# Moving the z sums of a linear attention to another PSUM bank and slot, and one gate step in the layer behind it

## The chip, the cores and the metric

The kernel runs on one core of a Trainium2 chip. The metric is the device time of one execution in microseconds. The kernel before takes 821.87 us, the median of three runs (821.83 to 821.92).

## The reference

The work is a linear attention, then a gated layer, then a layer of eight experts of which each token takes one. Constants of shape: 4 batches, 8 heads, 576 positions, 64 channels a head, 128 features; 2304 tokens of 512 channels; hidden widths 2048 and 1024.

```python
def phi(x):                                   # 64 -> 128 -> 256 features
    proj = x @ w_phi
    proj = proj - max(abs(proj), axis=-1)
    return concatenate([exp(proj), exp(-proj)], axis=-1)
q_p, k_p = phi(q), phi(k)
kv = k_p.T @ v                                # per head, 256 x 64
z = sum(k_p, axis=positions)                  # per head, 256
x = (q_p @ kv) / (q_p @ z + 1e-6)             # numerators, denominators

h = x @ w_in                                  # 2304 x 2048
g = h * clip(h + 3, 0, 6) / 6
x = g @ w_out

e = argmax(x @ w_gate)                        # one of 8 experts a token
out = gate * sigmoid(x @ w_output_gate)[e] * (relu(x @ w1[e]) @ w2[e])
```

## The kernel before

Everything is one program with an instruction list written out by hand for each engine; the engines meet in semaphores. Nothing is planned at build time: the order of the calls in the functions below is the order of the work.

**Attention** takes the 32 heads in 16 pairs. Each engine has a function `both(u, a)` for pair `u` (`a` is its parity, for double buffers), unrolled for the first and last pairs and looped between; `last_pair` ends it. From the eighth pair on (the second half, `phase` 1) ScalarE and VectorE also scale the pieces of w_in and w_out into two float16 parts; before that, VectorE searches them for their maximum. The steps of a pair are:

- TensorE projects q and k tiles of the next pair in three groups (`projections`, line 749: tiles of 64 rows; group 0 is one tile, groups 1 and 2 are four).
- VectorE searches maxima, subtracts them for q and negates them for k (`differences`).
- ScalarE makes the exponentials of k (`k_features`, line 1144) and, behind TensorE's transposes (line 765), those of q (`q_features`, line 1127).
- TensorE sums kv over positions into PSUM bank KVB (line 781), ScalarE copies it (`copy_kvt`, line 1156), TensorE turns it (`kv_transposes`, line 790), ScalarE copies it again (`copy_kv`, line 1162).
- GpSimd adds the k features of all tiles (`sums_first`, `sums_second`, lines 596 and 612), five additions; its result `pk_summed` goes to TensorE's `z_sums` (line 799: four tiles of 32 columns), then ScalarE's `copy_z_rows` (line 1168), TensorE's `z_transpose` (line 805), ScalarE's `copy_z` (line 1174).
- TensorE makes the low and high numerators (line 812, tiles of 64 columns, banks NB and NB + 1) and the denominators (line 821, tiles of 32 columns, both banks). ScalarE copies the low bank (`copy_low`, lines 1180 and 1181), VectorE the high one (`copy_high`).
- The denominators go through DRAM to get turned and spread: SP issues `den_over`, VectorE takes reciprocals, SP issues `rec_out` and `rec_in`, GpSimd multiplies (`normalise`, line 616).

The banks: KVB is 0, NB is 6, KB is (3, 5). In the kernel before z rows and z stand in bank KVB behind kv. In two pairs (`top`) a maximum over partitions is also found (`max_turn`, `max_over`, lines 828 and 832).

SP's queue issues the loads of q and k (`next_qk`), of v (`next_v`, four DMAs), of weight pieces (`next_pieces`, two DMAs) and the three steps of the denominators, in the order of the loop at line 454. A step that waits holds up all that are behind it.

**The gated layer** takes the tokens in 6 blocks of 384, and each block in 16 column chunks `f` of the hidden width. Per chunk: TensorE's `hidden` (line 925, 12 matmuls), ScalarE's relu (line 1284), VectorE's product (`gate_chunk`, line 1684), ScalarE's high half of the gate (line 1295, semaphore `g_hi`), VectorE's low half (`gate_lo`, line 1689, semaphore `g_ready`), TensorE's `output` (line 936, 9 matmuls). TensorE works two chunks ahead: `hidden(f + 2)`, then `output(f)`. Between these steps VectorE and ScalarE prepare the expert weights in units: per unit VectorE searches four quarters for their maximum in two steps (line 1606), reduces it (line 1610), GpSimd reduces over partitions (line 646), VectorE makes the scale (lines 1621 to 1624), ScalarE scales the quarters (line 1272), VectorE makes their low halves (line 1631). In `mlp_block` of VectorE the first unit's second search is at chunk 3, its scale at chunk 4, its first low halves at chunk 5. In ScalarE's `mlp_block` the first quarter follows the gate's half of chunk 4 and stands ahead of the relu of chunk 5; the second follows that relu, ahead of the wait for the product.

Where `gate_lo` of a chunk stands is set by one line: for chunks in `SOON` it comes right behind `gate_chunk`, for all others at the end of the chunk's work:

```python
SOON = (0, 1, 2, FC - 1)            # line 69, FC = 16
...
gate_chunk(n, f)                    # lines 1732 to 1734
if f in SOON:
    gate_lo(n, f)
...
if j == 2 and 0 <= k < units:       # line 1757, k, j = divmod(f - 1, 5)
    unit_search(n * 3 + k, (a + k) % 2, 2)
...
if f not in SOON and not (post and f == Y_AT + 9 - ahead):
    gate_lo(n, f)                   # line 1775
```

**The experts** follow in slots of 128 tokens (lines 1026 and 1038).

## Time and profile before

| | us |
|---|---|
| median of three runs | 821.87 |
| profiled execution | 821.83 |
| its span | 820.2 |
| attention, to about | 182 |
| gated layer, to about | 563 |

```profile
PE 802.9 (98%) x7080; PEld 498.6 (61%) x7081; DVE 558.2 (68%) x1144; ACT 390.8 (48%) x863; POOL 182.7 (22%) x210
PE   9999999999999999999999999999999999999995
DVE  6788798878988988988898897845723453222221
ACT  6888888884655654754645646534101121010110
POOL 4456666660000011010010001010311232111000
PEclk9999999999999999999999999999999999999998
PE 58%; DVE 18%; issue 12%; ACT 8%; DMA 2%; POOL 1%; DVEq 0%; POOLq 0%; ACTq 0%
```

The first line gives each engine's busy time, its share of the span and its instructions. PE is TensorE's matmuls, PEld its loads of weights, which overlap them, DVE is VectorE, ACT ScalarE, POOL GpSimd. The next lines cut the span into 40 equal slices of 20.5 us; a digit is the busy share in tenths, and for PEclk the granted clock of TensorE. Attention is the first nine slices, the gated layer goes to slice 27. The last line is the chain that ended last, by engine. A busy TensorE means that matmuls were in flight, not that they ran at their best rate.

### The profile page before, as it was taken

The page shows a single profiled execution, that of the slowest core. Times are in us where ns is not written, and L with a number is a line of the kernel's source. Part 1 is how long each engine was busy: PE and PEld are TensorE (multiplying, and loading weights), DVE is VectorE, ACT ScalarE, POOL GpSimd, SP SyncE. Part 2 cuts the span into 40 slices and gives each one's busy share as a digit, 9 for nine tenths or more (in the row PEclk, how much of TensorE's full clock was granted, in tenths as well). Part 3 has the DMA queues.
Part 4 walks back from the last instruction along what each step waited for, and adds up shares of the span by engine and source line. Part 5 has one row for each costly group of instructions (what it writes and reads, how often), then busy time and mean ns, then how long its engine had stood idle before and what let it go on. Part 6 is the DMA issues. An engine that isn't in the chain of part 4 may idle for free.

```text
span 820.2 us, 19346 instructions
## 1 busy us (share of the span) xinstructions
PE 802.9 (98%) x7080; PEld 498.6 (61%) x7081; DVE 558.2 (68%) x1144; ACT 390.8 (48%) x863; POOL 182.7 (22%) x210
## 2 busy tenths in 40 slices
PE   9999999999999999999999999999999999999995
PEld 7666666655555555555555555556777777777773
DVE  6788798878988988988898897845723453222221
ACT  6888888884655654754645646534101121010110
POOL 4456666660000011010010001010311232111000
PEclk9999999999999999999999999999999999999998
DMA  8566778736557657765765766394274926166600
GB/s 254 182 199 219 213 202 243 217 110 220 220 205 225 225 216 237 240 227 208 218 246 179 245 217 198 135 343 145 85 278 164 361 64 256 61 242 240 237 27 15
DMA packets 67454, 164.41 MB, mean 200 GB/s; under 512 B 28614, under 2 KB 32966, under 8 KB 60736
## 3 DMA queue, kind: packets, MB, share of 16 engines
q1 hardware_dynamic: 61472, 146.74, 52.9%
q0 software_dynamic: 5760, 16.80, 5.8%
q8 instruction: 36, 0.59, 0.3%
q14 instruction: 26, 0.21, 0.1%
q10 hardware_dynamic: 160, 0.07, 0.0%
HBM read 114.16 MB, written 47.55 MB: 197 GB/s over the span
## 4 chain that ended last, share of the span: by engine, by line
PE 58%; DVE 18%; issue 12%; ACT 8%; DMA 2%; POOL 1%; DVEq 0%; POOLq 0%; ACTq 0%
PE ps L936 11%; PE ps L1026 11%; PE ps L1038 11%; PE ps L925 10%; DVE u_mx L1606 4%; DVE arena L1631 4%; PE ps L749 3%; ACT arena L1144 3%; PE ps L781 3%; DVE relu L1684 2%; PE ps L812 2%; DVE y_words L1598 2%; DVE arena L1356 1%; DVE stage L1689 1%; PE ps L765 1%
## 5 line engine op out<-in xcount | busy, mean ns | idle before, releaser
L925 PE MATMUL ps<-arena,w_in_sb 128*128 128x384 f16 x1152 | 200.9, 326 | 0.0
L936 PE MATMUL ps<-w_out_sb,arena 128*128 128x512 f16 x576 | 171.3, 379 | 1.8 <-DVE stage L1689 1.8
L925 PEld LDWEIGHTS ps<-arena,w_in_sb 128*128 128x128 f16 x1152 | 111.9, 98 | 81.1 <-issue 0.2
L1323 ACT ACTIVATE x_t<-ps 128x512 f16<-128x512 f32 x54 | 31.6, 596 | 198.7 <-PE ps L1026 173.4
L1026 PE MATMUL ps<-x_t,arena 128*128 128x128 f16 x2112 | 121.5, 219 | 1.3 <-issue 1.3
L1026 PEld LDWEIGHTS ps<-x_t,arena 128*128 128x128 f16 x2112 | 119.2, 98 | 5.1 <-issue 1.8
L1038 PE MATMUL ps<-arena,x_t 128*128 128x512 f16 x528 | 117.9, 379 | 0.0
L936 PE MATMUL ps<-w_out_sb,stage 128*128 128x512 f16 x288 | 109.1, 379 | 0.0
L1295 ACT ACTIVATE arena<-relu 128x384 f16<-128x384 f32 x96 | 50.0, 521 | 122.6 <-DVE relu L1684 122.4
L936 PEld LDWEIGHTS ps<-w_out_sb,arena 128*128 128x128 f16 x576 | 55.9, 98 | 61.8 <-issue 4.6
L1797 DVE SCALAR_TENSOR_TENSOR x_t<-ps,x_t 128x512 f16<-128x512 f32 x54 | 36.7, 689 | 77.8 <-ACT x_t L1323 77.8
L1144 ACT ACTIVATE arena<-ps,arena 128x128 f32<-128x128 f32 x288 | 81.5, 416 | 9.7 <-DVE arena L1353 9.7
L1038 PEld LDWEIGHTS ps<-arena,x_t 128*128 128x128 f16 x528 | 50.6, 98 | 56.7
L596 POOL TENSOR_TENSOR arena<-arena 128x512 f32<-128x512 f32 (+1 forms) x64 | 69.2, 1081 | 59.6 <-ACT arena L1144 55.5
L1631 DVE SCALAR_TENSOR_TENSOR arena<-arena,u_up 128x1024 f16<-128x1024 f32 x64 | 79.3, 1280 | 3.7 <-ACT arena L1272 3.7
L1284 ACT ACTIVATE relu<-ps,three,s_h 128x384 f32<-128x384 f32 x96 | 63.5, 662 | 38.0 <-PE ps L925 37.4
L1272 ACT ACTIVATE arena<-arena,u_up 128x1024 f16<-128x1024 f32 x64 | 72.5, 1140 | 6.2 <-DVE u_up L1623 6.2
L1606 DVE TENSOR_REDUCE u_mx<-arena 128x1 f32<-128x1024 f32 x64 | 74.8, 1210 | 0.0
L646 POOL PARTITION_ALL_REDUCE u_all<-u_red x16 | 7.8, 490 | 290.9 <-DVE u_red L1610 290.9
L1684 DVE SCALAR_TENSOR_TENSOR relu<-relu,ps 128x384 f32<-128x384 f32 x96 | 52.7, 549 | 26.3 <-ACT relu L1284 24.6
L1807 DVE TENSOR_SCALAR x_t<-ps,stage 128x512 f32<-128x512 f32 x27 | 20.2, 748 | 68.5 <-PE ps L1038 68.5
L1689 DVE SCALAR_TENSOR_TENSOR stage<-relu,arena 128x384 f16<-128x384 f32 x96 | 53.1, 553 | 19.4 <-ACT arena L1295 19.2
(210 smaller groups left out, 912.8 us busy)
## 6 DMA issues: line engine op xcount, KB each, us to landing
arena<-split SPq DMA_DIRECT2D x36, 1024.0 KB
arena<-in_moe_w SPq DMA_DIRECT2D x16, 2048.0 KB, 12.8
split<-arena SPq DMA_DIRECT2D x16, 2048.0 KB, 7.4
arena<-in_qkt SPq DMA_DIRECT2D x15, 576.0 KB, 4.2
stage<-in_moe_w_in SPq DMA_DIRECT2D x16, 512.0 KB, 4.4
stage<-in_moe_w_out SPq DMA_DIRECT2D x16, 512.0 KB, 5.7
x_t<-rows POOLq DMA_DIRECT2D x27, 257.0 KB
y_words<-recs SPq DMA_DIRECT2D x32, 144.0 KB, 3.9
```

The lines of the kernel that those rows point to most:

```text
L596: nc.gpsimd.tensor_tensor(out, x, y, ALU.add).then_inc(sum_step, 1)
L925: last = nc.tensor.matmul(ps[:, HB[f % GB], 0:BN], w_in_sb[:, lw, c, f * P:(f + 1) * P], xt[:, a, lx, c, :], start=c == 0 and lw + lx == 0 ...
L936: last = nc.tensor.matmul(ps[:, YB + r, :], g_sb[lg_][:, f % GB, r * P:(r + 1) * P], w_out_sb[:, lw, f, :], start=f == 0 and lg_ + lw == 0 ...
L1026: last = nc.tensor.matmul(ps[:, bank, f % 4 * P:(f % 4 + 1) * P], w1_sb[b][:, lw, c, f * P:(f + 1) * P], xgt[:, a, lx, c, :], start=c == 0 ...
L1038: last = nc.tensor.matmul(ps[:, 6 + a, :], hg[:, a, lh, f, :], w2_sb[b][:, lw, f, :], start=f == 0 and lh + lw == 0, stop=f == EFC - 1 and ...
L1144: last = nc.scalar.activation(pk[:, t0 + t, s, :], ps[:, bank, t * F:(t + 1) * F], ACT.Exp, bias=bias[:, t0 + t:t0 + t + 1], scale=1.0 - 2 ...
L1272: nc.scalar.activation(split_sb[:, 0, q_ * Q:(q_ + 1) * Q], raw[b][:, q_ * Q:(q_ + 1) * Q], ACT.Copy, scale=u_up[:, b:b + 1]).then_inc(u_h ...
L1284: nc.scalar.activation(relu3[:, f % GB, :], ps[:, HB[f % GB], 0:BN], ACT.Relu, bias=three[:, 0:1], scale=s_h[:, 0:1]).then_inc(relu3_ready, 1)
L1606: nc.vector.tensor_reduce(u_mx[:, q_:q_ + 1], raw[b][:, q_ * Q:(q_ + 1) * Q], AX.X, ALU.max, apply_absolute_value=True).then_inc(u_searche ...
L1631: nc.vector.scalar_tensor_tensor(out=split_sb[:, 1, cols], in0=raw[b][:, cols], scalar=u_up[:, b:b + 1], in1=split_sb[:, 0, cols], op0=ALU ...
L1684: nc.vector.scalar_tensor_tensor(out=relu3[:, f % GB, :], in0=relu3[:, f % GB, :], scalar=6.0, in1=ps[:, HB[f % GB], 0:BN], op0=ALU.min, o ...
L1689: nc.vector.scalar_tensor_tensor(out=g_sb[1][:, f % GB, :], in0=relu3[:, f % GB, :], scalar=CG / 6.0, in1=g_sb[0][:, f % GB, :], op0=ALU.m ...
```

## The change

In attention the z rows and z move from bank KVB to bank NB + 1 (in the last pair to bank 3), which the high numerators overwrite. TensorE makes the z sums ahead of the low numerators, turns z right behind them, and waits for the copy of z ahead of the high numerators; the wait of the denominators goes. ScalarE's `both` has k features of group 0 ahead of `copy_kv` and `copy_low`, and makes both z copies before the next pair's k features of group 1, no longer in their midst. SP issues values and reciprocals ahead of the weight pieces, and reciprocals one pair sooner. In the gated layer chunk 3 joins `SOON`.

```diff
--- before.py
+++ after.py
@@ -66,7 +66,7 @@
 USTEPS = 4
 Y_AT = 3
 UNIT_AT = 1
-SOON = (0, 1, 2, FC - 1)
+SOON = (0, 1, 2, 3, FC - 1)
 W_UP = 3
 YSTEPS, YUP = 6, 4
 ONEHOT, ARGS, ROUTE = 7, 9, 19
@@ -332,11 +332,12 @@
 
 
         QB, KB, TB, KVB, NB = 4, (3, 5), (1, 2), 0, 6
-        DEN_AT, ZR_AT, Z_AT = LOW, 2 * F, 2 * F + P
+        DEN_AT, ZR_AT, Z_AT = LOW, 0, F
         TOPS, MAX_AT = (PAIRS // 2 - 1, PAIRS - 2), DEN_AT + QUARTER
         KQ, RUN = (1, 0), (7, 6)
         FIRST = (TB[::-1], (NB, NB + 1), (QB, KB[0]))
         WEIGHTS, VALUES = (0, 3), (1, 1)
+        Z_LAST = KB[0]
 
         YB, HB, XB, LB = 0, (3, 4, 5), 6, 7
         TURNED, AHEAD = (6, 7, 1, 4), 2
@@ -452,14 +453,14 @@
 
             next_qk(2)
             for u in range(PAIRS):
-                if u > 3:
-                    rec_in(u - 4)
                 if u > 2:
                     rec_out(u - 3)
+                if u + 2 < PAIRS:
+                    next_v(u + 2)
+                if u > 2:
+                    rec_in(u - 3)
                 if 0 < u < PAIRS - 1:
                     next_pieces(u - 1)
-                if u + 2 < PAIRS:
-                    next_v(u + 2)
                 if u > 0:
                     den_over(u - 1)
                 if u + 3 < PAIRS:
@@ -484,7 +485,6 @@
                 sp.dma_start(split[bass.ds(e, 1), m, :, :].rearrange("o p n -> (o p) n"),
                              split_sb.rearrange("p l n -> p (l n)")).then_inc(u_stored, 16)
 
-            rec_in(PAIRS - 4)
             sp.wait_ge(num_done, PAIRS)
             load_unit(0, 0, 0)
             rec_out(PAIRS - 3)
@@ -790,19 +790,21 @@
                     last = nc.tensor.transpose(ps[:, KVB, s * P:s * P + P], kvt_sb[:, s, :], ident[:])
                 last.then_inc(kv_transposed, 1)
 
-            def z_sums(u):
+            def z_sums(u, bank=NB + 1):
 
                 pe.wait_ge(pk_summed, u + 1)
+                if bank == NB + 1 and (not isinstance(u, int) or u > 0):
+                    pe.wait_ge(high_copied, u)
                 for s in range(2):
                     for hh in range(2):
                         g = REP * (2 * s + hh)
-                        last = nc.tensor.matmul(ps[g:g + REP, KVB, ZR_AT:ZR_AT + F], ones[:, 0:REP], pk_sum[:, hh, s, :],
+                        last = nc.tensor.matmul(ps[g:g + REP, bank, ZR_AT:ZR_AT + F], ones[:, 0:REP], pk_sum[:, hh, s, :],
                                                 start=True, stop=True)
                 last.then_inc(z_summed, 1)
 
-            def z_transpose(u):
+            def z_transpose(u, bank=NB + 1):
                 pe.wait_ge(zr_ready, u + 1)
-                nc.tensor.transpose(ps[:, KVB, Z_AT:Z_AT + P], zr_sb, ident[:]).then_inc(z_turned, 1)
+                nc.tensor.transpose(ps[:, bank, Z_AT:Z_AT + P], zr_sb, ident[:]).then_inc(z_turned, 1)
 
             def numerators(bank, k, n, signs=(0, 1)):
 
@@ -841,20 +843,20 @@
                 dif_transposes(u, a, 2)
                 kv_transposes(u)
                 projections(u + 1, 1 - a, 1)
+                z_sums(u)
                 pe.wait_ge(kv_ready, u + 1)
                 pe.wait_ge(pq_ready, u * 3 + 2)
                 if not isinstance(u, int) or u > 0:
                     pe.wait_ge(low_copied, u)
                 numerators(NB, 0, LOW)
-                z_sums(u)
+                z_transpose(u)
                 projections(u + 1, 1 - a, 2)
-                z_transpose(u)
+                if top == VALUES:
+                    max_turn(*top)
                 pe.wait_ge(pq_ready, u * 3 + 3)
-                if not isinstance(u, int) or u > 0:
-                    pe.wait_ge(high_copied, u)
+                pe.wait_ge(z_ready, u + 1)
                 numerators(NB + 1, LOW, HIGH)
-                pe.wait_ge(z_ready, u + 1)
-                if top is not None:
+                if top == WEIGHTS:
                     max_turn(*top)
                 last = denominators()
                 if top is not None:
@@ -875,11 +877,11 @@
                 pe.wait_ge(low_copied, u)
                 numerators(NB, 0, LOW)
                 pe.wait_ge(pk_ready, u * 3 + 3)
-                z_sums(u)
+                z_sums(u, Z_LAST)
                 pe.wait_ge(pq_ready, u * 3 + 3)
                 pe.wait_ge(high_copied, u)
                 numerators(NB + 1, LOW, HIGH, (0,))
-                z_transpose(u)
+                z_transpose(u, Z_LAST)
                 numerators(NB + 1, LOW, HIGH, (1,))
                 pe.wait_ge(z_ready, u + 1)
                 denominators().then_inc(num_done, 1)
@@ -1129,7 +1131,7 @@
                                                 scale=1.0 - 2.0 * s)
                 last.then_inc(pq_ready, 1)
 
-            def k_features(u, a, g, between=None):
+            def k_features(u, a, g):
                 t0, n = GROUPS[g]
                 act.wait_ge(neg_ready, u * 3 + (g + 1))
                 if g == 0 and (not isinstance(u, int) or u > 0):
@@ -1145,8 +1147,6 @@
                                                     bias=bias[:, t0 + t:t0 + t + 1], scale=1.0 - 2.0 * s)
                     if g == 2 and t == 2:
                         last.then_inc(pk_half, 1)
-                    if between is not None and t == 1:
-                        copy_z(between)
                 last.then_inc(pk_ready, 1)
 
             def copy_kvt(u):
@@ -1161,17 +1161,17 @@
                     act.wait_ge(num_done, u)
                 nc.scalar.copy(kv_sb[:].rearrange("p s n -> p (s n)"), ps[:, KVB, 0:2 * P]).then_inc(kv_ready, 1)
 
-            def copy_z_rows(u):
+            def copy_z_rows(u, bank=NB + 1):
                 act.wait_ge(z_summed, u + 1)
                 if not isinstance(u, int) or u > 0:
                     act.wait_ge(z_turned, u)
-                nc.scalar.copy(zr_sb, ps[:, KVB, ZR_AT:ZR_AT + F]).then_inc(zr_ready, 1)
-
-            def copy_z(u):
+                nc.scalar.copy(zr_sb, ps[:, bank, ZR_AT:ZR_AT + F]).then_inc(zr_ready, 1)
+
+            def copy_z(u, bank=NB + 1):
                 act.wait_ge(z_turned, u + 1)
                 if not isinstance(u, int) or u > 0:
                     act.wait_ge(num_done, u)
-                nc.scalar.copy(z_sb[:].rearrange("p s h n -> p (s h n)"), ps[:, KVB, Z_AT:Z_AT + P]).then_inc(z_ready, 1)
+                nc.scalar.copy(z_sb[:].rearrange("p s h n -> p (s h n)"), ps[:, bank, Z_AT:Z_AT + P]).then_inc(z_ready, 1)
 
             def copy_low(u, a):
                 act.wait_ge(num_done, u + 1)
@@ -1203,13 +1203,14 @@
                 q_features(u, 0)
                 q_features(u, 1)
                 copy_kvt(u)
+                k_features(u + 1, 1 - a, 0)
+                copy_kv(u)
                 if not isinstance(u, int) or u > 0:
                     copy_low(u - 1, 1 - a)
-                copy_kv(u)
-                k_features(u + 1, 1 - a, 0)
+                copy_z_rows(u)
                 q_features(u, 2)
-                copy_z_rows(u)
-                k_features(u + 1, 1 - a, 1, between=u)
+                copy_z(u)
+                k_features(u + 1, 1 - a, 1)
                 if phase:
                     piece_hi_of(u, a)
 
@@ -1226,8 +1227,8 @@
                 copy_low(u - 1, 0)
                 copy_kv(u)
                 q_features(u, 2)
-                copy_z_rows(u)
-                copy_z(u)
+                copy_z_rows(u, Z_LAST)
+                copy_z(u, Z_LAST)
                 piece_hi_of(u, 1)
                 copy_low(u, 1)
                 nc.scalar.activation(wg_sb[:, 0], wg_raw[:], ACT.Copy, scale=s_up[:, 2:3]).then_inc(wg_hi, 1)
```

## Rows read from the trace of the kernel before

**Rows 1.** The waits of TensorE: line, what it waited for, us, times, longest.
```profile
PE ps L936 <- DVE stage L1689: 1.8, 5, 0.6
```

**Rows 2.** Windows: length; busy PE, PEld, DVE, ACT, POOL (x count); clock; DMA share; GB/s.
```profile
67.08:77.75 10.67, 10.67 (x126) 6.80 (x124) 8.66 (x18) 8.71 (x30) 6.63 (x7) 1.00 0.66 214
111.28:122.20 10.92, 10.79 (x124) 6.80 (x125) 9.82 (x20) 9.69 (x32) 7.51 (x7) 1.00 0.80 229
```

**Rows 3.** Time line before denominators: start us, us, instruction [idle before <-releaser].
```profile
71.51 1.08 PE L812 MATMUL ps<-arena 128*64 128x256 f32 x8
...
71.94 0.28 ACT L1174 COPY arena<-ps 128x128 f32<-128x128 f32 x1
...
72.52 0.89 PEld L821 LDWEIGHTS ps<-arena 128*32 128x32 f32 x32 [0.39 <-ACT arena L1174]
```

**Rows 4.** The time line at the low numerators, first half.
```profile
66.98 1.27 POOL L612 TENSOR_TENSOR arena<-arena 128x512 f32<-128x512 f32 x1
...
68.54 1.30 PE L812 MATMUL ps<-arena 128*64 128x320 f32 x8
```

**Rows 5.** The waits of ScalarE, at the copy of z rows.
```profile
ACT arena L1168 <- PE ps L799: 12.9, 16, 0.8
```

**Rows 6.** The time line of the first pair.
```profile
14.32 1.27 POOL L612 TENSOR_TENSOR arena<-arena 128x512 f32<-128x512 f32 x1
...
15.16 1.30 PE L812 MATMUL ps<-arena 128*64 128x320 f32 x8
```

**Rows 7.** The time line of one pair of the second half.
```profile
111.28 0.20 PEld L790 LDWEIGHTS ps<-ident,arena 128*128 128x128 f32 x2 [0.37 <-ACT arena L1156]
...
111.65 1.16 PE L749 MATMUL ps<-wphi_sb,arena 64*128 64x128 f32 x16
...
115.12 1.14 ACT L1144 ACTIVATE arena<-ps,arena 128x128 f32<-128x128 f32 x4 [0.40 <-DVE arena L1353]
...
117.55 5.10 POOL L596 TENSOR_TENSOR arena<-arena 128x512 f32<-128x512 f32 x4 [3.10 <-ACT arena L1144]
...
122.72 1.27 POOL L612 TENSOR_TENSOR arena<-arena 128x512 f32<-128x512 f32 x1
```

**Rows 8.** The time line of block 1, chunks 2 to 4.
```profile
255.76 0.56 DVE L1689 SCALAR_TENSOR_TENSOR stage<-relu,arena 128x384 f16<-128x384 f32 x1 [0.59 <-ACT arena L1295]
...
261.40 0.55 DVE L1689 SCALAR_TENSOR_TENSOR stage<-relu,arena 128x384 f16<-128x384 f32 x1
261.66 0.49 POOL L646 PARTITION_ALL_REDUCE u_all<-u_red  x1 [26.56 <-DVE u_red L1610]
261.86 0.55 DVE L1684 SCALAR_TENSOR_TENSOR relu<-relu,ps 128x384 f32<-128x384 f32 x1
...
262.09 0.59 PE L936 MATMUL ps<-w_out_sb,arena 128*128 128x512 f16 x2 [0.26 <-DVE stage L1689]
...
263.59 1.15 ACT L1272 ACTIVATE arena<-arena,u_up 128x1024 f16<-128x1024 f32 x1 [0.63 <-DVE u_up L1623]
```

**Rows 9.** The time line at chunk 5 of blocks 0, 1, 2 and 5.
```profile
206.32 0.55 DVE L1689 SCALAR_TENSOR_TENSOR stage<-relu,arena 128x384 f16<-128x384 f32 x1
...
207.17 0.59 PE L936 MATMUL ps<-w_out_sb,arena 128*128 128x512 f16 x2
...
268.78 0.55 DVE L1689 SCALAR_TENSOR_TENSOR stage<-relu,arena 128x384 f16<-128x384 f32 x1
...
269.87 0.38 PE L936 MATMUL ps<-w_out_sb,arena 128*128 128x512 f16 x1
...
332.48 0.56 DVE L1689 SCALAR_TENSOR_TENSOR stage<-relu,arena 128x384 f16<-128x384 f32 x1
...
333.27 0.59 PE L936 MATMUL ps<-w_out_sb,arena 128*128 128x512 f16 x2
...
522.48 0.55 DVE L1689 SCALAR_TENSOR_TENSOR stage<-relu,arena 128x384 f16<-128x384 f32 x1
...
523.75 0.59 PE L936 MATMUL ps<-w_out_sb,arena 128*128 128x512 f16 x2
```

## The prediction

> **What bounds the kernel now.** I read three views, in this order. First the waits of TensorE: it is idle hardly anywhere, and the largest entry is five waits of up to 0.6 us for VectorE's line 1689, the low half of the gate [rows 1]. Then the windows over one head pair of attention: 10.67 us in the first half, 10.92 us in the second [rows 2]. TensorE is busy for all of the first and for all but 0.13 us of the second, so in attention it is the bound, or within 0.25 us of it. Last the time line around each place that the diff touches, to see how much earlier than needed each semaphore comes. The profiled execution took 821.83 us, with a span of 820.2 us; that is 0.04 under the median of 821.87, so I add the changes to 821.83 and call the rest the same.
>
> **The attention part, costs of the instructions.** No matmul, copy or activation is added or removed: the four z sums, the z transpose and their two copies move, to another bank and another place. TensorE shows a gap of 0.39 us ahead of the denominators' weights, for which it names the copy of z [rows 3]. If that gap were the wait, merging it into the one ahead of the high numerators would pay. But the copy ends at 71.94 + 0.28 = 72.22, 0.30 before the weights at 72.52. What the gap costs beyond the streaming: eight matmuls go in four couples from 71.51 to 72.59; with 0.38 for one, the last couple starts at 72.21 and the couples are 0.23 apart, so a next one was due at 72.44, 0.08 before 72.52. I count these 0.08 us as the price of going from 128x64 to 128x32 tiles, not of the wait. The order before has the shapes projection, numerators, z sums, projection, z transpose, numerators, denominators; the order after has projection, z sums, numerators, z transpose, projection, numerators, denominators: six changes each. So I take 0; the bounds are 0 and a gain of 16 x 0.08 = 1.3 us. The Trainium skill (TensorEngine Tiling (Array Packing), Key Properties) says that changing the tiling mode drains TensorE, while a change of tile alone does not. By it the sum stays at 0 here; by the other reading it would fall by 1.3 us.
>
> **The z sums now come 1.2 us earlier, and wait for GpSimd.** They stood behind the low numerators; now they take the numerators' slot, right behind the second projections. That slot opens at 68.54, 1.46 us behind the pair's start at 67.08 [rows 2, 4]. GpSimd ends the sums of features (line 612) at 66.98 + 1.27 = 68.25 [rows 4], so in the first half there is 0.29 us to spare. The other waits that move (for the low and high halves of the pair before, and for z) cost nothing there either: ScalarE stood idle for 0.8 us a pair at the z rows (12.9 us in 16 waits [rows 5]) and takes the copies into that time. So 0 for seven pairs; with that idle time gone, the low copy's pass would be late by at most as much.
>
> Not so in the first pair. GpSimd ends its sum at 14.32 + 1.27 = 15.59, the slot opens at 15.16 [rows 6]. With 0.07 us for the semaphore the z sums start at 15.66: **+0.50 us**. TensorE is the bound behind it, so this is not given back. Bounds 0.3 to 0.6.
>
> **Second half.** What ends last is now ScalarE: TensorE idles before the kv transposes for the copy of kv (the 0.37) [rows 7], which is the 0.25 us between the two windows [rows 2]. ScalarE's loop is k features, z copy, a weight piece, more k and q features, kv copy. The z copy leaves it for ScalarE's idle time. It has a duration of 0.28 us [rows 3], but the queue's instructions overlap; I take half, 0.14, bounds 0 and 0.28. ScalarE's loop would then allow 10.92 - 0.14 = 10.78 us.
>
> But the z sums need GpSimd. From the second projections of a pair (111.65 [rows 7]) to the first activation of the next pair's k features (115.12) are 3.47 us; from there to GpSimd's start (117.55) 2.43, now 2.29 without the z copy; GpSimd's five additions take from 117.55 to 122.72 + 1.27 = 123.99, which is 6.44 us; the semaphore 0.07. So z sums of a pair start no earlier than 12.27 us behind the second projections of the pair before. And from the z sums to the next pair's second projections TensorE needs 10.67 us less the way from projections to slot, 1.46 - 0.37 = 1.09 (0.37 is 111.28 to 111.65), so 9.58 us. Two pairs therefore take at least 12.27 + 9.58 = 21.85 us, **10.93 us a pair**, against 10.92 before. The wait for kv goes and a wait for GpSimd of about 0.25 us at the z sums takes its place. With the entry into this phase I take **+0.1 us** for the half. Bounds: -1.0 (seven times 0.14, GpSimd not binding) and +3.1: GpSimd works 7.51 us in a pair of this half and 6.63 in one of the first [rows 2], 0.88 more, because one of its additions meets a VectorE pass over a weight piece; a second meeting would cost two pairs 0.88, one pair 0.44, seven pairs 3.1. The Trainium skill (GPSIMD Engine Reference, Specifications) has GpSimd's memory interface in contention with VectorE instructions with two SBUF inputs. That is the kind of pass meant here, so it bears on the upper bound alone.
>
> **The DMA queue.** SP now issues the values' four loads and the two loads of reciprocals ahead of the two weight pieces. The pieces so leave later by six issues. A piece is read by VectorE only in the second pair behind its issue, so a whole pair, 10.67 us [rows 2], lies between; 0. If that lead were gone, VectorE would stand at a piece, and the projections behind it.
>
> **The gated blocks: line 69 (SOON).** For column chunk 3 of each block the low half of the gate is made right behind the product, no longer behind VectorE's second search of a weight unit. These are the five waits of rows 1, each at chunk 3 of blocks 1 to 5. At the old place it ran at once, 261.40, and kept VectorE 0.46 us until the next product at 261.86. At the new one it has to wait for ScalarE's half, which starts only when the product is done: in chunk 2, where this order already stands, VectorE idles 0.59 and works 0.56 [rows 8], 1.15 us together. All that follows is late by 1.15 - 0.46 = **0.69 us**, and that is the unit's scale (line 1621). GpSimd's maximum, which the scale also needs, is there at 261.66 + 0.49 = 262.15, 1.44 before ScalarE's first quarter at 263.59 [rows 8]; between them lie only VectorE's product and its own short steps, so it does not hide the delay.
>
> From the scale on it is a chain without slack: ScalarE's first quarter waits for the scale (0.63 us idle for line 1623) [rows 8], its relu of chunk 5 stands behind that quarter, VectorE's product behind the relu, ScalarE's next quarter, VectorE's two passes over quarters, and last the low half of chunk 5. So the latter is late by 0.69 us. TensorE's output matmul starts 0.14 us behind the end of such a half when it waits for it (261.40 + 0.55 = 261.95, then 262.09) [rows 8]. That gives, for chunk 5 [rows 9]:
> block 0: 206.32 + 0.55 + 0.69 + 0.14 = 207.70, before 207.17: +0.53;
> block 1: 268.78 + 0.55 + 0.83 = 270.16, before 269.87: +0.29; block 3 has the same distances;
> block 2: 332.48 + 0.56 + 0.83 = 333.87, before 333.27: +0.60; block 4 likewise;
> block 5: 522.48 + 0.55 + 0.83 = 523.86, before 523.75: +0.11.
> The removed wait at chunk 3 is already in these: TensorE arrives earlier at chunk 5 and waits there instead. Sum 0.53 + 2 x 0.29 + 2 x 0.60 + 0.11 = **+2.42 us**. From chunk 6 on the halves come early enough. Bounds: +2.9 (0.1 us more in each of five blocks) and, without the chain, the -1.8 us of the waits [rows 1].
>
> **Sum.** 0.50 + 0.1 + 2.4 = 3.0 us: 821.83 + 3.0 = **824.8 us**.
>
> **The rivals.**
> *A, faster: the delay ends before TensorE.* Place: chunk 5. If VectorE's later work absorbs the 0.69 us, only the removed waits at chunk 3 count, -1.8 us, and with the first pair +0.5 and the second half between -1.0 and +0.1 the time is 819.5 to 820.6. It decides as soon as the low half of chunk 5 is late by less than 0.2 us in block 0 and on time in block 2, since these have no slack: in block 0 the half ends at 206.87, and 0.14 later is 0.16 before the start at 207.17. For it: the waits of rows 1 are real. Against it: no idle time in the chain that I can find but the ones counted.
> *B, GpSimd does not bind:* ScalarE's 10.78 rules, second half -1.0: 823.7. Or the gap before the denominators was the wait, -1.3: 823.5. For it: 0.15 us a pair decides between the loops. Against: by the sum above GpSimd ends 0.5 us behind the slot at the shorter rhythm (12.27 against 10.67 + 1.09 = 11.76).
> *C, GpSimd meets VectorE twice:* +3.1, 827.9.
> *D, parts cancel:* half of A's effect, the time within 1.6 us of before.
>
> **How the numbers follow.** Chances: my forecast 0.58 (own range 824.0 to 826.0), B 0.13, C 0.05, A 0.16, D 0.08. 0.2% is 1.64 us, about what can be told from no change. Faster by more than that needs A with the better attention, and A's edge lies on it: 0.15. D and the rest of A: 0.11. Slower: 0.74. The range 820.7 to 826.4 leaves out A's better half and C, and a little on each side.
>
> **What would show it.** In the trace of after: the z sums of the first pair idle until GpSimd at 15.66; pairs of 10.67 us, then of 10.93, with the wait for the kv copy gone and one for line 612 in its place; no wait at chunk 3, but five or six at chunk 5 that name line 1689, of 0.3 to 1.0 us; the denominators' gap as before. I am wrong on the sign if chunk 5 shows none, and wrong in the attention part if the pairs of the second half take 10.8 us or less.

## The result: slower by 0.7%, and the profile after

| | before | after |
|---|---|---|
| median of the executions timed side by side, us | 821.83 | 825.88 |
| spread of these five | 820.69 to 821.92 | 824.88 to 828.56 |
| ratio, 95% interval | | 1.0069 (1.0046 to 1.0094) |
| profiled execution, us | 821.83 | 828.33 |
| its span, us | 820.2 | 826.7 |
| attention, to about | 181.8 | 184.8 |
| gated layer, its length | 381.1 | 384.1 |
| experts, their length | 247.5 | 248.0 |

The kernel after is slower, by 3.8 to 7.7 us (the interval times 821.83). Its executions lie further apart than those of before: with the profiled one and two more (829.33 and 829.37) the median of all eight is 827.6, and the ratio fits these eight. The profiled one lost 3.0 us in attention, 3.0 in the gated layer and 0.5 behind it.

The page after: busy time, VectorE and granted clock in 40 slices, and the chain that ended last.

```profile
PE 802.4 (97%) x7080; PEld 497.4 (60%) x7081; DVE 557.6 (67%) x1144; ACT 394.2 (48%) x863; POOL 183.6 (22%) x210
DVE  6788789877978988898897897845622453222221
PEclk9999999999999999999999999999999999999998
PE 53%; DVE 21%; issue 11%; ACT 5%; DMA 5%; POOL 3%; SPq 1%; DVEq 0%; ACTq 0%; POOLq 0%
```

The matmuls take what they took (802.4 us against 802.9) at the same clock, so the loss is idle time of TensorE. The chain shows whose: DMA has grown from 2% to 5% of it, VectorE from 18% to 21%. TensorE's waits name the places (line, what it waited for, us, times, longest); the first answers to [rows 1], the others had no row among them:

```profile
PE ps L938 <- DVE stage L1690: 4.5, 7, 1.1
PE ps L834 <- DVE s_row L1437: 2.4, 2, 1.7
PE ps L801 <- POOL arena L612: 1.4, 6, 0.4
PE ps L790 <- ACT arena L1156: 0.7, 2, 0.3
```

Lines have moved by a few: 938 is the output, 1690 the gate's low half, 834 the maximum over partitions, 801 the z sums, 790 the kv transposes. The windows over one pair of the first half, one of the second, and the last two full pairs (length; busy PE, PEld, DVE, ACT, POOL; clock; DMA share; GB/s) answer to [rows 2]:

```profile
67.02:77.67 10.65, 10.65 (x127) 6.80 (x125) 8.68 (x18) 8.96 (x31) 6.63 (x7) 1.00 0.69 205
122.07:132.96 10.89, 10.71 (x126) 6.80 (x124) 9.54 (x19) 10.01 (x32) 7.50 (x7) 1.00 0.72 227
154.77:166.23 11.46, 10.91 (x126) 6.76 (x124) 9.40 (x19) 10.03 (x32) 8.06 (x7) 1.00 0.67 208
166.23:179.75 13.52, 11.16 (x125) 6.88 (x125) 10.30 (x21) 9.90 (x32) 9.23 (x8) 1.00 0.60 171
```

Behind the first pair the windows have the lengths that were forecast, 10.65 and 10.89, up to 154.77. Then two pairs take 0.5 and 2.6 us more than the 10.92 they took before: this is the loss in attention. The chain of waits through them (start us, us, what; a wait on a transfer stands at its issue):

```profile
154.87 7.71 DMA recs<-rec
162.59 0.46 SPq L434
...
163.74 0.58 SPq L396
...
164.36 7.57 DMA stage<-in_moe_w_out
171.93 0.02 issue
171.95 0.76 DVE w_in_sb L1420
```

SP stores the reciprocals at 154.87, and the next step in its queue is now the load of the same reciprocals (`rec_in(u - 3)`, line 434). It stands there until the store has landed, 7.71 us, with the two weight pieces behind it. They are issued at 163.74 and 164.36, and the later one lands at 171.93, when VectorE has been standing at it for 1.9 us (the other 0.8 us of the row belong to the pair before):

```profile
DVE w_in_sb L1420 <- DMA stage<-in_moe_w_out: 2.7, 2, 1.9
```

In the trace of before, SP issued the same two right behind the store:

```profile
152.39 0.33 SPq L417 DMA_DIRECT2D recs<-rec  x1
154.30 0.34 SPq L395 DMA_DIRECT2D stage<-in_moe_w_in  x1
154.68 0.44 SPq L398 DMA_DIRECT2D stage<-in_moe_w_out  x1
```

In the gated layer the time line of block 1, chunks 2 to 4, answers to [rows 8]:

```profile
261.98 0.55 DVE L1685 SCALAR_TENSOR_TENSOR relu<-relu,ps 128x384 f32<-128x384 f32 x1
...
263.12 0.56 DVE L1690 SCALAR_TENSOR_TENSOR stage<-relu,arena 128x384 f16<-128x384 f32 x1 [0.59 <-ACT arena L1296]
...
267.80 1.15 ACT L1273 ACTIVATE arena<-arena,u_up 128x1024 f16<-128x1024 f32 x1 [0.63 <-DVE u_up L1624]
```

Chunk 3's low half (263.12) idles VectorE for 0.59 us as foreseen. ScalarE's first quarter starts at 267.80, against 263.59 before. VectorE's products up to chunk 3 are 3.49 us behind the trace of before, so the quarter is 267.80 - 263.59 - 3.49 = 0.72 us late; 0.69 was forecast. Chunk 5 of blocks 0, 1 and 2 [rows 9], and chunk 15 of block 1:

```profile
210.66 0.59 PE L938 MATMUL ps<-w_out_sb,arena 128*128 128x512 f16 x2 [0.37 <-DVE stage L1690]
...
273.69 0.59 PE L938 MATMUL ps<-w_out_sb,arena 128*128 128x512 f16 x2 [0.58 <-DVE stage L1690]
...
309.70 0.59 PE L938 MATMUL ps<-w_out_sb,arena 128*128 128x512 f16 x2 [0.18 <-DVE stage L1690]
...
338.13 0.59 PE L938 MATMUL ps<-w_out_sb,arena 128*128 128x512 f16 x2 [1.02 <-DVE stage L1690]
```

The row at 309.70 had not been foreseen. Pairing the 96 outputs and the 96 VectorE products (line 1685) of both traces in order gives how far each is behind the trace of before, in us:

| block | TensorE at its end | VectorE's products, chunks 4 to 15 | chunk 5 added (forecast) | chunk 15 added |
|---|---|---|---|---|
| 0 | 3.49 | 3.64, then 3.49 from chunk 11 | 0.53 (0.53) | 0 |
| 1 | 4.15 | 4.20 to 4.22 | 0.32 (0.29) | 0.34 |
| 2 | 4.86 | 4.92 to 4.95 | 0.71 (0.60) | 0 |
| 3 | 5.73 | 5.79 to 5.81 | 0.53 (0.29) | 0.34 |
| 4 | 6.33 | 6.38 to 6.45 | 0.60 (0.60) | 0 |
| 5 | 5.97 | 7.02, then 6.45 from chunk 9 | 0.11 (0.11) | -0.48 |

"Added" is net of the wait at chunk 3 that goes. The two columns sum to 2.80 and 0.20, and 2.95 (attention) + 3.00 is the 5.97 at the end, within rounding. In blocks 1 to 4 VectorE does not catch up once in twelve chunks: it hands its lateness on.

### The profile page after: what moved, and what is told of

It is laid out like the page before. It is cut to its first block, busy times and chain, and to the rows that moved or that the text cites. A ratio compares the mean times of both kernels' runs of the same rounds, so it can differ in the third digit from the quotient of the medians.

```text
span 826.7 us, 19359 instructions
## 1 busy us (share of the span) xinstructions
PE 802.4 (97%) x7080; PEld 497.4 (60%) x7081; DVE 557.6 (67%) x1144; ACT 394.2 (48%) x863; POOL 183.6 (22%) x210
## 4 chain that ended last, share of the span: by engine, by line
PE 53%; DVE 21%; issue 11%; ACT 5%; DMA 5%; POOL 3%; SPq 1%; DVEq 0%; ACTq 0%; POOLq 0%
PE ps L1028 11%; PE ps L1040 11%; PE ps L938 10%; PE ps L927 9%; DVE u_mx L1607 5%; DVE arena L1632 4%; DMA recs<-rec 3%; PE ps L749 2%; DVE relu L1685 2%; PE ps L781 2%; PE ps L814 2%; DVE stage L1690 2%; POOL arena L596 2%; ACT arena L1296 2%; DMA stage<-in_moe_w_out 2%
## 5 line engine op out<-in xcount | busy, mean ns | idle before, releaser
L596 POOL TENSOR_TENSOR arena<-arena 128x512 f32<-128x512 f32 (+1 forms) x64 | 71.0, 1109 | 60.1 <-ACT arena L1146 55.9
L1146 ACT ACTIVATE arena<-ps,arena 128x128 f32<-128x128 f32 x288 | 79.1, 399 | 7.8 <-DVE arena L1354 7.8
```

The costliest lines, as they stand in the source:

```text
L596: nc.gpsimd.tensor_tensor(out, x, y, ALU.add).then_inc(sum_step, 1)
L1146: last = nc.scalar.activation(pk[:, t0 + t, s, :], ps[:, bank, t * F:(t + 1) * F], ACT.Exp, bias=bias[:, t0 + t:t0 + t + 1], scale=1.0 - 2 ...
```

## The experiments

Each is compared with executions of the kernel before on the same chip (medians 821.56 to 821.81). The diffs are against the kernel named.

**Three parts, taken apart.** First the kernel after with SyncE's old order:

```diff
+                if u > 3:
+                    rec_in(u - 4)
                 if u > 2:
                     rec_out(u - 3)
-                if u + 2 < PAIRS:
-                    next_v(u + 2)
-                if u > 2:
-                    rec_in(u - 3)
                 if 0 < u < PAIRS - 1:
                     next_pieces(u - 1)
+                if u + 2 < PAIRS:
+                    next_v(u + 2)
...
+            rec_in(PAIRS - 4)
```

> The kernel after, with SP's order of issues as before the change (weight pieces ahead of the values, reciprocals loaded four pairs behind). Theory 1 (the loss in attention comes from SP, which now waits in line for the store of reciprocals, 7.7 to 7.9 us, and so issues the last weight pieces 9.6 us late): pairs 14 and 15 return to 10.9 us or less, attention ends about 3 us sooner, 3 us less than after in all, near 824 us, and with little spread between runs. Theory 2 (the loss comes from the earlier maximum matmul of pair 14 or from the ordering of the z sums): pair 14 still waits 1.7 us for line 1437 and the time stays near that of after. The wait at chunk 5 stays in both.

Measured 825.53 (824.51 to 826.23), ratio 1.0052 (1.0038 to 1.0066). Attention ends at 181.2 in its trace, the gated layer takes 383.9. In the profiled executions the 3 us of attention come and go with SyncE's order. In the timings it was not yet told: 825.53 is more than the expected 824, the five times of after run from 824.88 up, the lowest lie among these, and the two intervals overlap.

The kernel after without `3` in SOON:

```diff
-SOON = (0, 1, 2, 3, FC - 1)
+SOON = (0, 1, 2, FC - 1)
```

> The kernel after, with chunk 3 out of SOON again. Theory 1 (low half of chunk 3 made early delays the low half of chunk 5 by 0.69 us): the six waits ahead of the output of chunk 5 go, five waits at chunk 3 of up to 0.6 us return, and the gated blocks are 2.4 to 3.0 us shorter than in after. Rival (the gated blocks are longer because weights or reciprocals arrive later from the new DMA order): the waits stay and the time too.

Measured 822.41 (820.78 to 825.36, 11 executions), ratio 1.0016 (1.0006 to 1.0026). The gated layer is back at 380.9, and attention, with SyncE's new order, ends at 181.6.

The kernel before with `3` in SOON and nothing else:

> The kernel before, with chunk 3 in SOON and nothing else. Theory 1: +2.4 us by the sum of the prediction, up to +3.0 by the trace of after; waits of 0.3 to 1.0 us ahead of the output of chunk 5 in all six blocks. Rival (it costs only together with the rest of the change): between -1.8 and 0.

Measured 824.65 (824.24 to 825.12), ratio 1.0039 (1.0026 to 1.0053): +3.2 us, 2.1 to 4.4. The gated layer takes 383.9. TensorE's wait is that of after:

```profile
PE ps L936 <- DVE stage L1689: 4.6, 8, 1.0
```

The kernel before with SyncE's new order and nothing else:

> The kernel before, with SP's order of issues as after and nothing else. Theory 1: about +3 us, all of it in pairs 13 to 15, with the last weight pieces issued 8 to 10 us later than before and VectorE waiting for them; more spread between runs, since the store's round trip varies. Theory 2 (SP's order is harmless without the moved z sums): within 0.5 us of before.

Measured 821.74 (820.64 to 822.76, 11 executions), ratio 1.0001 (0.9992 to 1.001). SyncE waits 40.4 us for its stores (49.9 in after, below), and it costs nothing here. That SyncE's order adds 3 us whenever it is there has fallen with this run. What was left: it costs only where the weight pieces come so late that their lead is used up, which happens in some executions and not in others.

```profile
SPq L433 <- DMA recs<-rec: 40.4, 11, 7.9
```

**The bank and the order on TensorE and ScalarE alone** (the change without its edits to SyncE and SOON):

> The kernel before with the first part of the change alone: the z tensors in their own bank, z sums and z transpose moved forward on TensorE, and ScalarE's copies moved with them. SyncE's order and SOON stay as before. My theory: this part is worth next to nothing. From the trace of after, the first pair costs 0.2 us, the six pairs of the second half take 10.90 us each instead of 10.92, and the first half 10.645 instead of 10.68 (6 x 0.035 = 0.2 us gained): sum about 0, time 821.4 to 822.0. The prediction had +0.6 (822.4). Rival: the part gains more and is hidden in after by the other two; then 820.8 to 821.2. In the list of waits, z sums <- GpSimd appears about six times with a mean of 0.4 us, and output <- VectorE with four or five of chunk 3, as before.

Measured 822.19 (821.7 to 824.6, 11 executions), ratio 1.001 (1.0001 to 1.0019): 0.1 to 1.6 us slower, between the two expectations, with the prediction's +0.6 inside. A window over a pair of the second half has the length of after, and in TensorE's waits the one for GpSimd is there six times:

```profile
133.03:143.96 10.93, 10.71 (x126) 6.81 (x124) 9.72 (x19) 9.97 (x32) 7.57 (x7) 1.00 0.83 230
```

```profile
PE ps L802 <- POOL arena L613: 1.3, 6, 0.4
```

**The same with GpSimd's last addition cut short:**

```diff
-                nc.gpsimd.tensor_tensor(pk_sum[:], pk_sum[:], pk[:, 5:8:2], ALU.add).then_inc(pk_summed, 1)
+                nc.gpsimd.tensor_tensor(pk_sum[:, :, :, 0:8], pk_sum[:, :, :, 0:8], pk[:, 5:8:2, :, 0:8], ALU.add).then_inc(pk_summed, 1)
```

> The same kernel with GpSimd's fourth addition for the z sums cut to 8 of its columns (the denominators then leave out most of four of the nine feature tiles' last term). If z sums wait for GpSimd in the second half, as the prediction's first two terms have it, the wait of about 0.25 us over the fixed 0.2 us goes in each pair of the second half: period 10.64 to 10.70 instead of 10.90, 6 x 0.25 = 1.5 us, and 0.2 us in the first pair: 1.5 to 1.7 us under the kernel with this part alone. Rival: the kv copy, whose wait was 0.156 us a pair before, is late again behind it, or VectorE's queue sets the period; then 0 to 0.6 us under it.

The whole time, 831.85, is not to be compared: the denominators change, with them the routing, and the experts take 258.5 us instead of 247.8. Attention can be compared. A window over a pair of its second half takes 10.75 us. In the time line of the same pair GpSimd's last addition is done in 0.25 us, and TensorE waits for ScalarE at the kv transposes instead:

```profile
132.92:143.67 10.75, 10.75 (x125) 6.80 (x124) 9.64 (x20) 9.98 (x32) 6.47 (x7) 1.00 0.84 236
```

```profile
132.92 0.20 PEld L791 LDWEIGHTS ps<-ident,arena 128*128 128x128 f32 x2 [0.23 <-ACT arena L1157]
...
133.43 0.25 POOL L613 TENSOR_TENSOR arena<-arena 128x32 f32<-128x32 f32 x1
```

GpSimd cost 0.14 to 0.18 us a pair; of its wait of 0.25, 0.11 comes back at the kv transposes, which then wait for ScalarE. The expected 10.64 to 10.70 was missed, the rival's lower half as well: ScalarE's loop stands at 10.75, the 10.78 of the prediction.

**Chunk 3's low half between the two quarters of the second search**, in the kernel before:

```diff
+MID = 3
...
-            def unit_search(u, b, q0):
+            def unit_search(u, b, q0, between=None):
...
+                    if q_ == 2 and between is not None:
+                        between()
...
-                        unit_search(n * 3 + k, (a + k) % 2, 2)
+                        unit_search(n * 3 + k, (a + k) % 2, 2, (lambda: gate_lo(n, f)) if f == MID else None)
...
-                    if f not in SOON and not (post and f == Y_AT + 9 - ahead):
+                    if f not in SOON and f != MID and not (post and f == Y_AT + 9 - ahead):
```

> The kernel before with the low half of chunk 3's gate weights placed between the two quarters of the second unit search on VectorE, instead of behind it (before) or ahead of it (after). My theory: the 2.8 to 3.2 us that SOON costs come from the unit scale being late on ScalarE, which makes chunk 5 late; with half of the search still ahead of the wait, chunk 3 is in time and chunk 5 no later than before. Then the chunk-3 waits of blocks 1 to 5 go (0.40 + 0.09 + 0.41 + 0.12 + 0.48 = 1.5 us in the trace of before) and chunk 5 has its waits of before: 820.2 to 821.0. Rival (VectorE is simply full over these chunks, and what chunk 3 gains chunk 5 loses): 821.4 to 822.2, with chunk 5 waiting longer by what chunk 3 waits less.

Measured 821.70 (820.51 to 822.19, 11 executions), ratio 0.9998 (0.9989 to 1.0007). The rival's number. The waits at chunk 3 are gone and five others stand in their place: three at chunk 5 of blocks 2 to 4 (from the time line, the one of block 2) and two at chunk 15 of blocks 1 and 3.

```profile
PE ps L937 <- DVE stage L1692: 1.6, 5, 0.6
```

```profile
333.64 0.59 PE L937 MATMUL ps<-w_out_sb,arena 128*128 128x512 f16 x2 [0.45 <-DVE stage L1692]
```

In the profiled execution the gated layer gains 0.65 us of the 1.5, less than the timings can tell. In block 1 VectorE's product of chunk 4 falls back by 0.03 us here, against 0.71 in after. So the same low half, made before the scale but without VectorE's idle 0.59 us, costs nothing: the 3 us are the price of the idle time on VectorE's queue, handed down. The rival's reason, that chunk 5 loses what chunk 3 gains, holds for the waits: 1.8 us in 5 before [rows 1], 1.6 us in 5 in the row above.

**Both together:**

> The first part of the change and the placing of chunk 3 between the quarters together, SyncE's order of before. If the parts add, this is the time of the first part alone less what the placing gains on the kernel before: 820.0 to 821.0 by my theory, 821.4 to 822.2 if the placing gains nothing.

Measured 821.65 (821.02 to 823.4, 11 executions), ratio 1.0003 (0.9994 to 1.0012). No version here beats the kernel before.

**SyncE's wait, settled.** Four kernels on one chip. After, once more:

> The changed kernel once more, beside the three others, for the spread of its time. Theory (a): part of its cost, 0 to 4 us, comes only in executions in which SyncE's wait for a reciprocal's store pushes the weight pieces out so far that VectorE stands at one; then the times lie spread from 824.5 to 829.5 with a median 0.5 to 2 us above the kernel with SyncE's old order. Rival (b): the first two sets of runs only differed by chip; then both have one median, 825.5, and one spread.

Measured 828.57 (826.57 to 830.12, 6 executions), ratio 1.0078 (1.0063 to 1.0093). In this trace too VectorE stands at weight pieces (2.6 us in 2 waits), and the last two full pairs take 11.85 and 12.09 us. After with SyncE's old order, once more:

> The changed kernel with SyncE's order of before, once more, on the chip of the others. (a): 824.5 to 826.3, median 825.3, and no wait for a weight piece. (b): the times of the changed kernel.

Measured 826.03 (824.82 to 826.76), ratio 1.0048 (1.0035 to 1.0061). The rival (b), one median for both, has fallen. Theory (a) had put after 0.5 to 2 us above this kernel; it is 2.5 us, and all but the lowest of its six times lie above the highest here. After, with the load back of a pair earlier:

```diff
-                if u > 2:
-                    rec_in(u - 3)
+                if u > 3:
+                    rec_in(u - 4)
...
+            rec_in(PAIRS - 4)
```

> The changed kernel, but the load of the reciprocals back is that of pair u - 4 instead of u - 3, at the place where the change put it. It then never follows on its own fresh store in SyncE's queue, so SyncE has nothing of 7 to 8 us to wait for, and the pieces are issued when a buffer is free. (a): the list of SyncE's waits has no load-back <- store row of over 1 us, the last piece is issued near 165 to 168 us instead of 171 to 175, and the time is that of SyncE's old order: 824.5 to 826.3, without the ones above. Rival (c): moving v ahead of the pieces by itself pushes them late; then some executions still lie above 827.

Measured 826.19 (824.62 to 826.25), ratio 1.0047 (1.0034 to 1.006). Theory (a) holds in what it says of the cause: 2.4 us below after, none above 826.25, and the same time as with the old order. Rival (c), with times above 827, did not show. But the value loads ahead of the pieces are not free. They wait for TensorE's sums of kv, and the pieces wait behind them (waits of SyncE from 100 to 185 us here; 0.6 us in one wait in before):

```profile
SPq L389 <- PE ps L782: 11.4, 6, 2.7
```

The pieces that leave at 154.30 in before leave at 159.19 here, 3.8 us later when counted from TensorE's kv transposes of that pair. And where the first half meets the second, VectorE stands 0.8 us at a piece (line 1412): this pair takes 12.45 us here and 11.93 in before. SyncE's waits for its stores, in after and here:

```profile
SPq L434 <- DMA recs<-rec: 49.9, 13, 8.1
```

```profile
SPq L434 <- DMA recs<-rec: 20.8, 7, 8.5
```

SyncE's time line here, last piece:

```profile
164.32 0.33 SPq L418 DMA_DIRECT2D recs<-rec  x1
164.76 1.29 SPq L434 DMA_DIRECT2D y_words<-recs  x2
166.19 0.49 SPq L396 DMA_DIRECT2D stage<-in_moe_w_in  x1
```

The last piece leaves 1.87 us behind the store, at 166.19, where after has it at 174.79. One thing was not as expected: a row over 1 us remains (7 waits, up to 8.5); within the second half it is 1.4 us in 4 waits.

With `3` out of SOON as well:

> The same with chunk 3 out of SOON as well: the bank part and SyncE's new order without its wait. What is left of the change when both of its costs are out. By the sum of the parts 821.5 to 822.4, no faster than the kernel before; if the bank part has a gain that the other two hid, 820.5 to 821.3.

Measured 823.05 (821.21 to 824.27, 11 executions), ratio 1.0015 (1.0006 to 1.0023): 0.5 to 1.9 us slower than before, and more than the expected 821.5 to 822.4. By its interval it could be the bank part's +0.1 to +1.6 alone. Its trace shows more: the pair between the halves takes 12.52 us instead of 11.93, with VectorE late at a piece as in the kernel above, and the last full pair 11.94 instead of 10.92, with 1.0 us ahead of the maximum's matmul for which no view names a cause.

## Why the prediction was right or wrong

**The direction was right, and so were the mechanisms of three terms; the term of the DMA queue, put at 0, had its mechanism wrong, and that of the gated blocks was too small.** 824.8 was forecast in a range to 826.4. The five executions side by side have their median at 825.88, the ratio puts it at 827.5, and the six of the repeated run have 828.57.

**The DMA queue: the step that failed.** The prediction counted the issues ahead of the pieces ("later by six issues") and the lead of a whole pair, and wrote 0. It had priced what SyncE issues and not what SyncE waits for: with `rec_in(u - 3)` behind `rec_out(u - 3)`, every iteration contains a wait of one store's way, 7.7 us, ahead of the pieces. They left 9.7 us later in the profiled execution (164.36 against 154.68) and were under way for 7.57 us instead of 5.42, and this used up the lead. Its own condition, "if that lead were gone, VectorE would stand at a piece", is what the trace shows.

The wait could not have been priced from the trace of before alone, since the new order made the store itself slower. These are all 16 stores of the reciprocals in before (KB each, median us from issue to landing); in after their median is 7.0:

```profile
recs<-rec SPq DMA_DIRECT2D x16, 4.5 KB, 3.2
```

In after, SyncE comes out of its wait and issues in one go two pieces of 512 KB (152.07 and 152.69), a load of q and k of 576 KB (153.87), a store of 257 KB (154.38) and right behind them this one (154.87), which lands 0.2 us behind the 257 KB. The kernel before with SyncE's new order alone has 6.3 us for these stores, and after with the old order 3.3, so it is the order that does it; that it does it by the large transfers ahead of the store is what the times suggest, and no run varies them alone. Some 3.8 us of the pieces' lateness stay when the load back comes a pair earlier; there the value loads' wait for TensorE stands ahead of the pieces.

The term costs 0 where the pieces just make it (the runs with SyncE's order alone, and without SOON) and up to about 3 us where two come late. By undoing the wait alone, the medians differ by 828.57 - 826.19 = 2.4 us. The two profiled executions behind this differ by 3.4 us: 1.7 in attention, but also 1.2 in the gated layer, which no wait for a piece explains; so how much of the 2.4 us lies at the pieces is not shown.

Why the executions differ is known in part. From pieces to pieces SyncE's round takes 11.9 and 11.7 us in after (140.18, 152.07, 163.74), TensorE's pair 10.9, so SyncE falls behind from pair to pair. In the two traces of the new order in which nothing is late, the stores of these rounds take 7.1 to 7.4 us (7.7 to 8.1 in after and its repeat), and the pieces leave at 161.39 and 161.16 instead of 163.74 and 164.37. Why the stores are quicker there is open: one of the two differs from after in SOON alone, which acts only behind attention. Of the 22 executions of these two kernels, two lie 2.5 and 3.6 us above the kernel before (824.28 and 825.36, both without SOON), so the loss may be there too and rarer.

**The gated blocks: +2.4 forecast, +3.0 in the trace, 3.2 (2.1 to 4.4) alone.** The delay of the scale was 0.72 for 0.69, and chunk 5 of blocks 0, 1, 4 and 5 came out to 0.03 us. What failed is the sentence that from chunk 6 on the halves come early enough. VectorE does not recover within blocks 1 to 4: 0.34 us more fall due at chunk 15 of blocks 1 and 3, VectorE starts blocks 2 and 3 0.07 and 0.22 us further behind than TensorE (which is most of what these two have over the forecast), and 0.48 come back at chunk 15 of block 5. Rival A, that VectorE absorbs the delay, is refuted by the same table.

**The first pair: +0.50 forecast.** +0.2 in the profiled execution of after, where the z sums began at 15.25. In the one of the repeated run they began at 16.30, and there it was 0.5: from its kv transposes to the next ones the first pair took 11.15 us (14.34 to 25.49), the pairs behind it 10.65.

```profile
14.98 1.26 POOL L612 TENSOR_TENSOR arena<-arena 128x512 f32<-128x512 f32 x1
...
16.30 0.42 PE L801 MATMUL ps<-arena,ones 128*32 128x128 f32 x8 [0.43 <-POOL arena L612]
```

Of the nine traces with the new order on TensorE and GpSimd's whole addition, five have 0.5 us, two have 0.2 and 0.3, and two have none (after with SyncE's old order, first run, and both parts together). The mechanism stands, the size changes with the execution; what sets it is not shown.

**The second half: right.** 10.93 us a pair forecast, 10.89 to 10.93 measured in the windows, with the kv wait replaced by one for GpSimd of 0.25 us. Rival C, a second meeting with VectorE, did not come (GpSimd busy 7.50 us a pair, 7.51 before [rows 2]). Rival B's 10.78 came as soon as GpSimd's addition was cut, at 10.75: the order of the two loops was read rightly, and it is the sum over GpSimd's path that decided it, by 0.14 to 0.18 us.

```profile
134.69 0.42 PE L801 MATMUL ps<-arena,ones 128*32 128x128 f32 x8 [0.19 <-POOL arena L612]
```

**The shapes: right, 0.** The gap ahead of the denominators stayed at 0.39 us, and the view names no releaser for it any more [rows 3]: it is not the wait for z.

```profile
72.43 0.89 PEld L823 LDWEIGHTS ps<-arena 128*32 128x32 f32 x32 [0.39 <-issue]
```

The first half even gains 0.03 us a pair (10.65 for 10.68), with the z sums now between two other shapes: 0.2 us in all, forecast at 0.

**Not settled.** The bank part alone is slower by 0.1 to 1.6 us in the timings, and its profiled execution equals that of before (821.81 against 821.83). The first pair's 0 to 0.5 is the only cost that a trace of this part shows, against 0.2 gained in the first half; where the rest is, if there is any, no run tells. With chunk 3 placed in the middle as well, the interval is -0.5 to +1.0 us.

## What to carry to other kernels

Before moving a step within an in-order DMA queue, write beside each step what it waits for and how long that takes, not how long its issue takes, and ask what will stand ahead of the transfer in the new order, for its duration in the old trace may not hold (3.2 us became 7.0 here); a load back of what the queue has just stored must not stand ahead of anything with a deadline. Where two engines run a chain with hardly any slack, follow a delay to the end of the block and into the next one: it is only over when the late engine has been seen idle. And a wait is worth what is left when the engine behind it has moved: all five of chunk 3 could be removed, and they came back at chunks 5 and 15.

## What the runs showed of the hardware

How long a small DMA takes changed here with the order of issues. The same store of 4.5 KB takes 3.2 us from issue to landing in the median of before and 7.0 in that of after, where it follows 1.9 MB issued within 3 us; in the two links of after's chain it takes 7.7 and 7.9 us, more than most of the 512 KB weight pieces (median 5.4 us, and 6.7 for the other kind, on the page):

```profile
recs<-rec SPq DMA_DIRECT2D x7, 4.5 KB, 7.4
...
stage<-in_moe_w_in SPq DMA_DIRECT2D x7, 512.0 KB, 5.5
```

These two rows are the transfers from 100 to 185 us, with the median from issue to landing. GpSimd's addition of 128x512 took 1.27 us alone and 2.14 beside a VectorE pass with two inputs over a weight piece; cut to 128x32 it took 0.25. Going from 64-column to 32-column tiles left a gap of 0.39 us on TensorE that is there with and without anything to wait for.
